# Sparse attention before two mixtures of experts: units of scores taken two by two, probabilities transposed a slot later, four buffers for them

## The chip, the cores and the metric

The kernel runs on one core of a Trainium2 chip. The metric is the device time of one execution in microseconds (us). Matrix work is done by TensorE (PE, with its weight loads listed as PEld), element-wise work by VectorE (DVE) and ScalarE (ACT), a little by GpSimd (POOL); SyncE (SP) issues most of the DMAs. PE writes only into PSUM (`ps`, eight banks of 512 float32 per partition), and DVE or ACT take results out of there.

## The reference, cut to what matters

Two batches, eight heads, 768 positions, head size 64. A position sees 8 global keys and the 96 keys up to itself, with a bias that falls with the distance. Behind it come a routed MoE (8 experts) and a dense one (4 experts).

```python
scores = scale * np.matmul(q, k.transpose(0, 1, 3, 2))
keep = is_global | is_local
bias = -slopes[:, None, None] * dist[None, :, :]
scores = np.where(keep, scores + bias, -1e9)
a = np.exp(scores - np.max(scores, axis=-1, keepdims=True))
a = a / (np.sum(a, axis=-1, keepdims=True) + 1e-09)
x = np.matmul(a, v)                       # then as (1536, 512)
# moe: rows with x @ w_skip > 0 go to expert argmax(x @ w_gate), others pass
# moe2: out = sum over e of p[:, e] * (relu(x @ w1[e]) @ w2[e])
```

## The kernel before, in words

The attention stage is the first 141 us. It has eight blocks `n` (`NB`; a pair of heads in one batch) of six units (`NI`; a tile of 128 queries), 48 units `u` in all. A query tile needs 256 keys: its own tile and a window made of the previous tile's last 96 keys and the first 32 keys of all; tile 0 needs its own 128 only and is the narrow unit. Each engine runs a program of its own, written out in order, and semaphores tie them; nothing is scheduled by a planner. So what stands behind a wait on its engine waits too.

For a unit the steps are these.

- `scores(u)` on PE: three products (high and low parts of float32 numbers, in fp32r), each for both heads, whose 64 rows lie in the two halves of the array. The result is in banks 0 and 1. It counts up `s_done`.
- `masked(u)` on DVE (L1080): adds the bias and takes the row's extreme, one instruction a head, into `p_sb` (one of three buffers) and `nmax`. `sm_done`.
- `exps(u)` on ACT (L805): the exponential in place, one a head. `ex_done`.
- `probs_T(u)` on PE (L1581): four transposes into bank 2 or 3. `pt_tr`.
- `probs_out(u)`: the copy of the transposed tile to SBUF, on ACT (L811) for tiles 1, 3 and 4 of a block (`by_act`), on DVE (L1089) for the others.
- `pv(u)` on PE (L1596, L1597): four float32 products with V and a column of ones, into bank 4 or 5. `pv_done`.

Beside the units a block has: four fills, which transpose keys and queries of the next block (`fill`, L1552) and of which ACT takes the high part (`keys_high`, `queries_high`, L785 and L791) and DVE the low part (`keys_low`, `queries_low`, L1058 and L1063); POOL's `windows`, which puts the key windows together (`kw_done`); `normalise` on DVE (L1096 to L1103), twice a block, for three tiles each; `outputs_T` on PE (L1605), which transposes the normalised outputs; `xo_out` on ACT (L797), their copy; `logits` on PE (L1613), their product with the router's weights; and `add_logits` on DVE (L1109).

In unit `u` PE's order is: scores(u), a fill for the next block, probs_T(u-1), in two units outputs_T, in two others logits, and pv(u-2). The logits of a half stand one unit behind the outputs_T of that half. The masks of unit `u` are made while PE transposes unit `u-1`. The fills and the transposed outputs share banks 6 and 7 in turn (`groups`, `group_bank`, `group_out`).

The stages behind the attention are not touched: routing, the first MoE (L1748), and the second (L1844 and L1867), which fills the last two thirds of the time. They start from the last addition of logits.

## Time and profile before

| | us |
|---|---|
| median of three runs | 780.96 (780.90 to 781.52) |
| the profiled execution, its own time | 780.86 |
| its span, first to last instruction | 779.1 |
| PE busy in the span | 752.0 (97%) |
| DVE busy | 471.3 (60%) |
| ACT busy | 328.7 (42%) |

The span is what the profiler sees from the first to the last instruction; the time lies 1.76 us above it. A timeline row gives start, duration, engine, source line, operation, output and inputs with their shapes, and how many instructions were merged in it; in brackets the idle time of the engine before it and what ended it. Merged rows of weight loads overlap each other, so starts tell more than durations. "issue" names idle time that no other engine is seen to end.

### The profile page before, as it was taken

The numbers are of one execution on the slowest core, as the hardware profiler recorded it, in microseconds if no ns is written. First come the engines' busy times: TensorE is split into PE (matmuls) and PEld (weight loads), VectorE is DVE, ScalarE is ACT, GpSimd is POOL, SyncE is SP. The second block draws the span as 40 slices with busy tenths as digits, with TensorE's granted clock in tenths as the row PEclk, the third lists the DMA queues.
The fourth block names the chain that finished last, engine by engine and source line by source line (L and its number), as shares of the span: only waits on it lengthen the run. The fifth ranks groups of instructions, "written<-read, shape, count | busy, mean of one in ns | idle before, by whom it ended". The sixth has DMA issues, their size and how long they took to land.

```text
span 779.1 us, 11259 instructions
## 1 busy us (share of the span) xinstructions
PE 752.0 (97%) x4199; PEld 671.5 (86%) x4199; DVE 471.3 (60%) x924; ACT 328.7 (42%) x586; POOL 42.0 (5%) x86
## 2 busy tenths in 40 slices
PE   3999999699999999999999999999999999999998
PEld 2889889488888988998989989989899899898896
DVE  5766666699888398554474375275365365456442
ACT  2566566388988263431422233234144053143230
POOL 3100100110100320000000000000000000000000
PEclk9999999699999999999999999999999999999999
DMA  9469970599990530020011011002003002000112
GB/s 151 100 151 263 274 218 21 204 393 389 390 389 25 163 117 5 1 109 0 1 55 55 1 54 55 1 4 105 0 0 108 0 0 109 0 0 0 40 40 81
DMA packets 86944, 79.28 MB, mean 102 GB/s; under 512 B 50802, under 2 KB 56948, under 8 KB 86900
## 3 DMA queue, kind: packets, MB, share of 16 engines
q1 hardware_dynamic: 81540, 71.32, 28.9%
q0 software_dynamic: 1600, 5.24, 2.1%
q10 hardware_dynamic: 3760, 2.14, 0.9%
q8 instruction: 26, 0.43, 0.2%
q14 instruction: 18, 0.15, 0.1%
HBM read 70.30 MB, written 8.39 MB: 101 GB/s over the span
## 4 chain that ended last, share of the span: by engine, by line
PE 91%; DVE 6%; DMA 1%; ACT 1%; issue 1%; POOL 0%; DVEq 0%; SPq 0%
PE ps L1867 32%; PE ps L1844 29%; PE ps L1748 11%; PE ps L1572 3%; PE ps L1597 2%; PE ps L1596 2%; PE ps L1581 2%; PE ps L1552 2%; PE ps L1799 1%; PE ps L1613 1%; PE ps L1804 1%; PE ps L1605 1%; PE ps L1723 1%; DVE xs L1441 1%; DVE X L1103 1%
## 5 line engine op out<-in xcount | busy, mean ns | idle before, releaser
L1867 PE MATMUL ps<-w2s,h_hi 128*128 128x512 f32 x768 | 237.1, 390 | 0.4 <-DVE X L1479 0.4
L1844 PE MATMUL ps<-xs,w1s 128*128 128x384 f32 x1344 | 236.6, 335 | 0.7 <-ACT xs L941 0.7
L1844 PEld LDWEIGHTS ps<-xs,w1s 128*128 128x128 f32 x1344 | 233.8, 188 | 2.2 <-ACT xs L941 0.9
L1867 PEld LDWEIGHTS ps<-w2s,h_hi 128*128 128x128 f32 x768 | 143.8, 188 | 29.9 <-DVE X L1479 0.8
L1867 PE MATMUL ps<-w2s,h_lo 128*128 128x512 f32 x384 | 149.8, 390 | 0.0
L1481 DVE SCALAR_TENSOR_TENSOR X<-ps,prn,X 128x512 f32<-128x512 f32 x84 | 63.1, 751 | 121.7 <-PE ps L1867 121.3
L951 ACT ACTIVATE shared<-ps 128x384 f32<-128x384 f32 x96 | 46.1, 488 | 156.2 <-PE ps L1844 156.0
L1450 DVE TENSOR_TENSOR shared<-ps,shared 128x384 f32<-128x384 f32 x96 | 53.3, 557 | 92.4 <-PE ps L1844 92.1
L1867 PEld LDWEIGHTS ps<-w2s,h_lo 128*128 128x128 f32 x384 | 72.1, 188 | 15.1
L954 ACT ACTIVATE h_hi<-shared 128x384 fp32r<-128x384 f32 x96 | 50.4, 526 | 67.8 <-DVE shared L1450 67.8
L1021 DVE TENSOR_TENSOR piece_lo<-ring,piece_hi 128x1024 fp32r<-128x1024 f32 x48 | 56.4, 1219 | 5.5 <-ACT piece_hi L773 5.4
L1080 DVE CUSTOM_DVE_ANT_0 area<-ps,shared 128x256 f32<-128x256 f32 (+1 forms) x96 | 34.8, 399 | 31.2 <-PE ps L1572 30.1
L1456 DVE SCALAR_TENSOR_TENSOR h_lo<-shared,h_hi 128x384 fp32r<-128x384 f32 x96 | 50.2, 551 | 2.0
L805 ACT ACTIVATE area<-area,shared 128x256 f32<-128x256 f32 (+1 forms) x96 | 41.6, 481 | 21.3 <-DVE shared L1080 21.3
L773 ACT ACTIVATE piece_hi<-ring 128x1024 fp32r<-128x1024 f32 x48 | 47.9, 1053 | 1.9 <-ACT area L888 1.9
L870 ACT ACTIVATE w2s<-raw 128x1024 fp32r<-128x1024 f32 x16 | 16.1, 1053 | 70.4 <-PE ps L1867 70.4
L1748 PE MATMUL ps<-piece_hi,xT_r 128*128 128x512 f32 x128 | 35.8, 402 | 0.8 <-ACT xT_r L883 0.8
L1597 PE MATMUL ps<-X,raw 128*128 128x65 f32 x192 | 35.8, 276 | 0.0
L1748 PE MATMUL ps<-piece_hi,hT_r 128*128 128x512 f32 x128 | 35.0, 396 | 0.0
L1596 PE MATMUL ps<-X,raw 128*128 128x65 f32 x160 | 30.0, 269 | 0.0
L1597 PEld LDWEIGHTS ps<-X,raw 128*128 128x128 f32 x192 | 28.9, 195 | 0.0
L1581 PE MATMUL ps<-ident,area 128*128 128x128 f32 x176 | 28.9, 284 | 0.0
(183 smaller groups left out, 819.5 us busy)
## 6 DMA issues: line engine op xcount, KB each, us to landing
ring<-in_moe_w SPq DMA_DIRECT2D x24, 1024.0 KB, 12.0
raw<-in_moe_w SPq DMA_DIRECT2D x16, 1024.0 KB, 5.1
shared<-in_moe_w SPq DMA_DIRECT2D x8, 1024.0 KB, 10.3
X<-in_k SPq DMA_DIRECT2D x16, 192.0 KB, 4.2
shared<-in_q SPq DMA_DIRECT2D x16, 192.0 KB, 4.3
X<-in_v SPq DMA_DIRECT2D x16, 192.0 KB, 2.9
x_d<-X SPq DMA_DIRECT2D x8, 384.0 KB, 3.2
X<-x_d SPq DMA_DIRECT2D x2, 1536.0 KB, 16.3
```

The costliest lines, as they stand in the source:

```text
L773: act.activation(unit(piece_hi[b % NHI], x), unit(piece_raw[b % NR], x), ACT.Copy).then_inc(p_hi, 1)
L951: act.activation(part[:, slot, f, :], ps[:, 3 * f + BANK[ITEMS[item][0]], 0:HT], ACT.Copy).then_inc(copied, 1)
L954: act.activation(h_hi[:, c, second * HT:second * HT + HT], src, ACT.Relu).then_inc(hd_hi, 1)
L1021: dve.tensor_tensor(unit(piece_lo[b % NR], x), unit(piece_raw[b % NR], x), unit(piece_hi[b % NHI], x).bitcast(F32), ALU.subtract).then_inc ...
L1450: dve.tensor_tensor(part[:, slot, f, :], ps[:, 3 * f + BANK[ITEMS[item][0]], 0:HT], part[:, slot, f, :], ALU.add).then_inc(added, 1)
L1456: dve.scalar_tensor_tensor(h_lo[c][:, here], src, 0.0, h_hi[:, c, here].bitcast(F32), ALU.max, ALU.subtract).then_inc(hd_lo, 1)
L1481: dve.scalar_tensor_tensor(X[:, t, :], ps[:, 6 + k % 2, :], p_, X[:, t, :], ALU.mult, ALU.add).then_inc(acc_done, 1)
L1596: pe.matmul(out_, pt_sb[u % 3][:, 2 * h, :], prev, start=True, stop=False)
L1597: mm = pe.matmul(out_, pt_sb[u % 3][:, 2 * h + 1, :], vn[b][:, i, h, :], start=(i == 0), stop=True)
L1748: mm = pe.matmul(ps[:, bank, :], src[xp][:, c0 + c, :], w[wp][:, c, :], start=(x == 0 and c == 0 and not (kind == "B" and half)), stop=(x ...
L1844: mm = pe.matmul(out_, w1s[:, wp, WI[name], c, f * P:(f + 1) * P], xs[:, 3 * b:3 * b + 3, xp, XI[name], c, :], start=(not onto and x == 0 ...
L1867: mm = pe.matmul(ps[:, 6 + k % 2, :], h_, w2s[:, wp, c, :], start=(x == 0 and c == 0), stop=(x == 2 and c == 3))
```

## The change

The program on PE, ACT and DVE goes by slots of two units `u` and `u+1`, three slots `s` a block. PE computes the scores of both one after the other; the second unit's result lies in the other half of banks 0 and 1 (`off`). Transposes of the probabilities are those of the slot before, as are their copies; P·V follows with unit `u-3` and `u-2`. There are four buffers of `p_sb` and `nmax`. `by_act` now means even units. Both fills of keys stand in slot 0, both fills of queries in slot 1. outputs_T of a block's first half and its xo_out stand in slot 0 of the next block and their logits in slot 1; outputs_T of the second half, its xo_out and its logits all stand in slot 2. The wait for `kw_done` moves from tile 0 to tile 1. DVE begins the masks of a slot when both scores are there, except in the first slot. `probs_T` and the index of `p_sb` in it change from `u % 3` to `u % 4` as in the other places. SP and POOL keep their programs.

Two places show what moves. The first is on PE, in the third block: around outputs_T of the second half (L1605, now L1615) of the block before. Scores are L1572, now L1582; probs_T L1581, now L1591; P·V L1596 and L1597, now L1606 and L1607; logits L1613, now L1623. Before:

```order
L1605 MATMUL ps<-ident,X 128x128 [waits o_done,q_lo]
L1605 MATMUL ps<-ident,X 128x128 x2
L1596 MATMUL ps<-X,raw 128x65 [waits pt_act]
L1597 MATMUL ps<-X,raw 128x65
L1596 MATMUL ps<-X,raw 128x65
L1597 MATMUL ps<-X,raw 128x65
L1572 MATMUL ps<-kh_52,qh_54 128x256 [waits sm_done,q_lo]
L1572 MATMUL ps<-kh_52,qh_54 128x256
L1572 MATMUL ps<-kh_52,ql_55 128x256 x2
L1572 MATMUL ps<-kl_53,qh_54 128x256 x2
L1581 MATMUL ps<-ident,area 128x128 [waits pt_act,ex_done]
L1581 MATMUL ps<-ident,area 128x128 x3
```

Now, from the last scores of slot 2 on:

```order
L1582 MATMUL ps<-kl_53,qh_54 128x256 x2
L1615 MATMUL ps<-ident,X 128x128 [waits o_done,q_lo]
L1615 MATMUL ps<-ident,X 128x128 x2
L1591 MATMUL ps<-ident,area 128x128 [waits pt_act,ex_done]
L1591 MATMUL ps<-ident,area 128x128 x3
L1606 MATMUL ps<-X,raw 128x65 [waits pt_dve]
L1607 MATMUL ps<-X,raw 128x65
L1606 MATMUL ps<-X,raw 128x65
L1607 MATMUL ps<-X,raw 128x65
L1591 MATMUL ps<-ident,area 128x128 [waits pt_dve,ex_done]
L1591 MATMUL ps<-ident,area 128x128 x3
L1623 MATMUL ps<-wg,area 128x9 [waits xo_cp]
```

outputs_T had the four transposes of probabilities in front of it and now comes first behind the scores. Before, the logits of that half followed behind the next unit's scores and transposes (just below the piece); now they stand in the same slot as their outputs_T.

The second place is on DVE, in the same block, tiles 2 and 3: queries_low (L1063, now L1069), normalise (L1096 to L1103, now L1102 to L1109), masked (L1080, now L1086) and probs_out (L1089, now L1095). Before:

```order
L1063 SCALAR_TENSOR_TENSOR ql_59<-ps,qh_58 128x512 [waits q_hi]
L1096 TENSOR_SCALAR shared<-ps 128x6 [waits pv_done]
L1098 RECIPROCAL shared<-shared 128x6 [waits o_step]
L1103 TENSOR_TENSOR X<-ps,shared 128x384 [waits o_step]
L1080 ISA area,shared<-ps,shared 128x256 [waits pt_tr,s_done]
L1080 ISA shared 128x1
L1080 ISA area,shared<-ps,shared 128x256
L1080 ISA shared 128x1
L1063 SCALAR_TENSOR_TENSOR ql_59<-ps,qh_58 128x256 [waits q_hi]
L1089 COPY raw<-ps 128x512 [waits pv_done,pt_tr]
```

Now:

```order
L1069 SCALAR_TENSOR_TENSOR ql_59<-ps,qh_58 128x512 [waits q_hi]
L1086 ISA area,shared<-ps,shared 128x256 [waits pt_tr,s_done]
L1086 ISA shared 128x1
L1086 ISA area,shared<-ps,shared 128x256
L1086 ISA shared 128x1
L1095 COPY raw<-ps 128x512 [waits pv_done,pt_tr]
L1069 SCALAR_TENSOR_TENSOR ql_59<-ps,qh_58 128x256 [waits q_hi]
L1102 TENSOR_SCALAR shared<-ps 128x6 [waits pv_done]
L1104 RECIPROCAL shared<-shared 128x6 [waits o_step]
L1109 TENSOR_TENSOR X<-ps,shared 128x384 [waits o_step]
```

normalise stood behind the first queries_low, ahead of masked for tile 3; it now stands behind that mask, a probs_out and the second queries_low.

```diff
@@ -157,10 +157,10 @@
             ql.append(take_r(f"ql{b}", NI, P))
         qn = [take(NI, 2 * D) for _ in range(2)]
         nbias = take(H, BW)
-        nmax = take(6)
+        nmax = take(8)
         rsum = take(6)
         rinv = take(6)
-        p_sb = [at(work, 512 * j, (4, P), "") for j in range(3)]
+        p_sb = [at(work, 512 * j, (4, P), "") for j in range(4)]
         Xf = X[:, :, :].rearrange("p t d -> p (t d)")
         vn = [at(Xf, 780 * b, (NI, 2, VW), "") for b in range(2)]
@@ -477,17 +477,19 @@
         NU_ = NB * NI
+        NS = NI // 2
         LG = 400
         FIRST = ["k0", "k1", "q0", "q1"]
-        FILL = FIRST + [None, None]
         groups = [(0, g) for g in FIRST]
         for n_ in range(NB):
-            for i_ in range(NI):
-                if n_ + 1 < NB and FILL[i_]:
-                    groups.append((n_ + 1, FILL[i_]))
-                if n_ and i_ in (0, 3):
-                    groups.append((n_ - 1, "xa" if i_ == 0 else "xb"))
+            for s_ in range(NS):
+                if n_ + 1 < NB and s_ < 2:
+                    groups += [(n_ + 1, g) for g in FIRST[2 * s_:2 * s_ + 2]]
+                if n_ and s_ != 1:
+                    groups.append((n_ - 1, "xb" if s_ else "xa"))
         groups += [(NB - 1, "xa"), (NB - 1, "xb")]
         place = {g: j for j, g in enumerate(groups)}
@@ -508,7 +510,7 @@
         def by_act(u):
-            return u % NI in (1, 3, 4)
+            return u % 2 == 0
         def pt_count(u):
@@ -801,8 +803,8 @@
                 c0 = 1 if u % NI == 0 else 0
                 for h in range(2):
                     act.wait_ge(sm_done, 2 * u + h + 1)
-                    part = p_sb[u % 3][:, 2 * h + c0:2 * h + 2, :]
-                    act.activation(part, part, ACT.Exp, bias=nmax[:, u % 3 * 2 + h:u % 3 * 2 + h + 1], scale=-1.0).then_inc(ex_done, 1)
+                    part = p_sb[u % 4][:, 2 * h + c0:2 * h + 2, :]
+                    act.activation(part, part, ACT.Exp, bias=nmax[:, u % 4 * 2 + h:u % 4 * 2 + h + 1], scale=-1.0).then_inc(ex_done, 1)
             def probs_out(u):
                 c0 = 1 if u % NI == 0 else 0
@@ -816,22 +818,26 @@
                     keys_high(0, c)
                 for c in range(2):
                     queries_high(0, c)
-                for u in range(NU_):
-                    n, i = u // NI, u % NI
-                    if n + 1 < NB and i < 4:
-                        if i < 2:
-                            keys_high(n + 1, i)
-                        else:
-                            queries_high(n + 1, i - 2)
+                for u in range(0, NU_, 2):
+                    n, s = u // NI, u % NI // 2
+                    high = (keys_high, queries_high, None)[s] if n + 1 < NB else None
+                    if high:
+                        high(n + 1, 0)
+                    if u:
+                        probs_out(u - 2)
                     exps(u)
-                    if n and i in (0, 3):
-                        xo_out(n - 1, i // 3)
-                    if u and by_act(u - 1):
-                        probs_out(u - 1)
-                    if n == NB - 1 and i < 2:
+                    if high:
+                        high(n + 1, 1)
+                    if n and s == 2:
+                        xo_out(n - 1, 1)
+                    exps(u + 1)
+                    if n and s == 0:
+                        xo_out(n - 1, 0)
+                    if n == NB - 1 and s < 2:
                         act.wait_ge(s_done, NI * (NB - 1))
                         piece_loaded(act, 0)
-                        piece_high(0, i)
+                        piece_high(0, s)
+                probs_out(NU_ - 2)
                 xo_out(NB - 1, 0)
                 xo_out(NB - 1, 1)
             with act.Else():
@@ -1073,14 +1079,14 @@
                     if i == 0 and n % 2 == 0:
                         dve.wait_ge(setup, 10 + 2 * (n // 2) + h)
                     if h == 0:
-                        dve.wait_ge(s_done, u + 1)
-                        wait(dve, pt_tr, u - 2)
+                        dve.wait_ge(s_done, u + 1 if u < 2 else u // 2 * 2 + 2)
+                        wait(dve, pt_tr, u - 3)
                     head = 2 * (n // 2) + h
                     lo = ONE if i == 0 else PREV
-                    dve.tensor_tensor_reduce(p_sb[u % 3][:, 2 * h + c0:2 * h + 2, :].rearrange("p a k -> p (a k)"),
-                                             ps[:, h, c0 * P:2 * P], nbias[:, head, lo:lo + (2 - c0) * P],
+                    dve.tensor_tensor_reduce(p_sb[u % 4][:, 2 * h + c0:2 * h + 2, :].rearrange("p a k -> p (a k)"),
+                                             ps[:, h, (u % 2 * 2 + c0) * P:(u % 2 * 2 + 2) * P], nbias[:, head, lo:lo + (2 - c0) * P],
                                              1.0, BIG, ALU.add, ALU.min,
-                                             accum_out=nmax[:, u % 3 * 2 + h:u % 3 * 2 + h + 1]).then_inc(sm_done, 1)
+                                             accum_out=nmax[:, u % 4 * 2 + h:u % 4 * 2 + h + 1]).then_inc(sm_done, 1)
             def probs_out(u):
                 c0 = 1 if u % NI == 0 else 0
@@ -1126,27 +1132,30 @@
                     queries_low(0, c)
                 for h in range(2):
                     head_bias(h)
-                for u in range(NU_):
-                    n, i = u // NI, u % NI
+                for u in range(0, NU_, 2):
+                    n, s = u // NI, u % NI // 2
+                    low = (keys_low, queries_low, None)[s] if n + 1 < NB else None
+                    if n and s == 0:
+                        normalise(n - 1, 0)
+                        if n > 1:
+                            add_logits(n - 2)
                     masked(u)
-                    if n + 1 < NB and i < 4:
-                        if i < 2:
-                            keys_low(n + 1, i)
-                        else:
-                            queries_low(n + 1, i - 2)
-                    if u and not by_act(u - 1):
+                    if low:
+                        low(n + 1, 0)
+                    masked(u + 1)
+                    if u:
                         probs_out(u - 1)
-                    if n and i == 2:
+                    if low:
+                        low(n + 1, 1)
+                    if n and s == 1:
                         normalise(n - 1, 1)
-                    if i == 5:
-                        normalise(n, 0)
-                        if n:
-                            add_logits(n - 1)
-                    if n == 0 and 2 + i < H:
-                        head_bias(2 + i)
+                    if n == 0:
+                        head_bias(2 + 2 * s)
+                        head_bias(3 + 2 * s)
+                normalise(NB - 1, 0)
+                add_logits(NB - 2)
                 unit_low(0, 0)
-                if not by_act(NU_ - 1):
-                    probs_out(NU_ - 1)
+                probs_out(NU_ - 1)
                 unit_low(0, 1)
                 normalise(NB - 1, 1)
                 add_logits(NB - 1)
@@ -1561,15 +1570,16 @@
             def scores(u):
                 n, i = u // NI, u % NI
                 b, c0 = n % 2, 1 if i == 0 else 0
-                if i == 0:
+                if i == 1:
                     pe.wait_ge(kw_done, 4 * n + 4)
                 if i in (0, 4):
                     pe.wait_ge(q_lo, 2 * n + i // 4 + 1)
-                wait(pe, sm_done, 2 * u)
+                wait(pe, sm_done, 2 * u if u < 2 else u // 2 * 4)
+                off = u % 2 * 2 * P
                 for x, (qt, kt) in enumerate(((qh, kh), (ql, kh), (qh, kl))):
                     for h in range(2):
                         r = slice(D * h, D * h + D)
-                        mm = pe.matmul(ps[:, h, c0 * P:2 * P], qt[b][r, i, :], kt[b][r, i, c0 * P:2 * P], start=(x == 0), stop=(x == 2))
+                        mm = pe.matmul(ps[:, h, off + c0 * P:off + 2 * P], qt[b][r, i, :], kt[b][r, i, c0 * P:2 * P], start=(x == 0), stop=(x == 2))
                 mm.then_inc(s_done, 1)
             def probs_T(u):
@@ -1618,21 +1628,33 @@
                 for g in FIRST:
                     fill(0, g)
                 pe.wait_ge(v_ones, 4)
-                for u in range(NU_):
-                    n, i = u // NI, u % NI
+                for u in range(0, NU_, 2):
+                    n, s = u // NI, u % NI // 2
                     scores(u)
-                    if n + 1 < NB and FILL[i]:
-                        fill(n + 1, FILL[i])
-                    if u >= 1:
+                    scores(u + 1)
+                    if n + 1 < NB and s < 2:
+                        for g in FIRST[2 * s:2 * s + 2]:
+                            fill(n + 1, g)
+                    if n and s == 1:
+                        logits(n - 1, 0)
+                    if n and s == 2:
+                        outputs_T(n - 1, 1)
+                    if u:
+                        probs_T(u - 2)
+                    if u >= 4:
+                        pv(u - 3)
+                    if u:
                         probs_T(u - 1)
-                    if n and i in (0, 3):
-                        outputs_T(n - 1, i // 3)
-                    if n and i in (1, 4):
-                        logits(n - 1, i // 3)
-                    if u >= 2:
+                    if n and s == 0:
+                        outputs_T(n - 1, 0)
+                    if n and s == 2:
+                        logits(n - 1, 1)
+                    if u:
                         pv(u - 2)
+                probs_T(NU_ - 2)
+                pv(NU_ - 3)
+                probs_T(NU_ - 1)
                 outputs_T(NB - 1, 0)
-                probs_T(NU_ - 1)
                 pv(NU_ - 2)
                 logits(NB - 1, 0)
                 pv(NU_ - 1)
```

## Rows read from the trace of the kernel before

**Rows 1.** Stages: stretch, length, busy us (instructions) by engine, PEclk, DMA share, GB/s.

```profile
60.00:80.00 20.00, 19.79 (x182) 18.11 (x182) 13.82 (x53) 12.52 (x31) 1.82 (x5) 1.00 0.95 278
...
136.00:138.00 2.00, 0.83 (x8) 0.73 (x7) 1.07 (x4) 0.00 (x0) 0.00 (x0) 0.93 0.00 0
138.00:140.00 2.00, 1.42 (x7) 1.02 (x6) 0.00 (x0) 0.49 (x1) 0.00 (x0) 0.50 0.62 191
```

**Rows 2.** Timeline, weight loads at two block beginnings: start, us, engine, line, what, count.

```profile
75.23 0.19 PEld L1572 LDWEIGHTS ps<-kh,qh 64*128 64x128 f32 x2
...
90.05 0.19 PEld L1572 LDWEIGHTS ps<-kh,qh 64*128 64x128 f32 x2
...
90.53 0.20 PEld L1552 LDWEIGHTS ps<-ident,X 128*128 128x128 f32 x2
```

**Rows 3.** Waits of the weight loads, 30 to 119 us: total, times, longest.

```profile
PEld ps L1605 <- issue: 2.5, 6, 0.4
```

**Rows 4.** Timeline, weight loads from 95 to 99 us.

```profile
95.00 0.30 PEld L1597 LDWEIGHTS ps<-X,raw 128*128 128x128 f32 x2
95.37 0.19 PEld L1572 LDWEIGHTS ps<-kh,qh 64*128 64x128 f32 x2
...
95.59 0.19 PEld L1572 LDWEIGHTS ps<-kl,qh 64*128 64x128 f32 x2
95.92 0.42 PEld L1552 LDWEIGHTS ps<-ident,shared 128*128 128x128 f32 x4
96.31 0.47 PEld L1581 LDWEIGHTS ps<-ident,area 128*128 128x128 f32 x4
...
98.94 0.31 PEld L1605 LDWEIGHTS ps<-ident,X 128*128 128x128 f32 x3 [0.42 <-issue]
```

**Rows 5.** Timeline, VectorE from 97 to 100 us.

```profile
97.24 0.69 DVE L1063 SCALAR_TENSOR_TENSOR ql<-ps,qh 128x512 fp32r<-128x512 f32 x1 [0.43 <-ACT qh L791]
97.85 0.15 DVE L1096 TENSOR_SCALAR shared<-ps 128x6 f32<-128x6 f32 x1
...
98.26 0.56 DVE L1103 TENSOR_TENSOR X<-ps,shared 128x384 f32<-128x384 f32 x1
...
99.08 0.42 DVE L1080 CUSTOM_DVE_ANT_0 area<-ps,shared 128x256 f32<-128x256 f32 x1
...
99.42 0.42 DVE L1063 SCALAR_TENSOR_TENSOR ql<-ps,qh 128x256 fp32r<-128x256 f32 x1
99.76 0.68 DVE L1089 COPY raw<-ps 128x512 f32<-128x512 f32 x1
```

**Rows 6.** Timeline, ScalarE from 96 to 99 us.

```profile
96.61 0.60 ACT L791 ACTIVATE qh<-ps 128x512 fp32r<-128x512 f32 x1 [1.69 <-PE ps L1552]
97.11 0.90 ACT L805 ACTIVATE area<-area,shared 128x256 f32<-128x256 f32 x2
97.91 0.58 ACT L811 ACTIVATE raw<-ps 128x512 f32<-128x512 f32 x1
98.38 0.38 ACT L791 ACTIVATE qh<-ps 128x256 fp32r<-128x256 f32 x1
```

**Rows 7.** Timeline at the end of the attention, ScalarE and weight loads.

```profile
138.76 0.49 ACT L797 ACTIVATE area<-ps 128x384 f32<-128x384 f32 x1 [4.39 <-PE ps L1605]
...
139.30 0.29 PEld L1613 LDWEIGHTS ps<-wg,area 128*128 128x128 f32 x1 [0.98 <-ACT area L797]
```

**Rows 8.** Timeline, a weight load and VectorE, last units of the attention.

```profile
133.29 0.31 PEld L1605 LDWEIGHTS ps<-ident,X 128*128 128x128 f32 x3 [0.54 <-issue]
...
140.79 0.21 DVE L1109 TENSOR_TENSOR lg<-ps,lg 128x54 f32<-128x54 f32 x1 [3.09 <-PE ps L1613]
```

**Rows 9.** Timeline, weight loads in the first block.

```profile
18.04 0.29 PEld L1572 LDWEIGHTS ps<-kh,qh 64*128 64x128 f32 x2 [0.33 <-DVE shared L1080]
...
18.98 0.29 PEld L1552 LDWEIGHTS ps<-ident,X 128*128 128x128 f32 x2 [0.22 <-issue]
...
20.67 0.29 PEld L1572 LDWEIGHTS ps<-kh,qh 64*128 64x128 f32 x2 [0.98 <-DVE shared L1080]
```

More of the change, by code:

```diff
@@ L1580, in probs_T @@
                     if u % NI or x % 2:
-                        mm = pe.transpose(ps[:, 2 + u % 2, x * P:(x + 1) * P], p_sb[u % 3][:, x, :], ident[:, :])
+                        mm = pe.transpose(ps[:, 2 + u % 2, x * P:(x + 1) * P], p_sb[u % 4][:, x, :], ident[:, :])
                 mm.then_inc(pt_tr, 1)
```

## The prediction

> **What bounds the kernel now.** I read the page first, then the stages, then the attention stage instruction by instruction, since the change touches nothing behind it. In a stretch of 20 us inside the attention TensorE (PE) is busy 19.79 us, VectorE (DVE) 13.82 and ScalarE (ACT) 12.52, at the full granted clock [rows 1]. So attention is bound by PE's own instructions, and nearly everything it waits for comes in time.
>
> The attention runs over eight blocks (a pair of heads of one batch each) of six units (query tiles). A block begins with the narrow scores of tile 0; two such beginnings stand at 75.23 and 90.05, so a block takes 14.82 us [rows 2]. The last addition of logits, the end of the attention, is at 140.79 [rows 8]. What stands behind it (routing, first MoE, second MoE) starts from there and is the same program, so what the attention gains or loses goes into the total one for one.
>
> Inside a block the only regular wait of PE is the one before L1605, the transposes of the normalised outputs: 2.5 us of weight-load idle in six waits between 30 and 119 us, 0.42 us each [rows 3]. The second cost that a reader should see is not called a wait anywhere: it is the edge between scores and everything else. Loads of one kind follow each other every 0.11 us: two of P·V, 0.19 each, fill 0.30 together from 95.00, so the last of them starts at 95.11. The first scores' load stands at 95.37, 0.26 behind it; the pairs of scores' loads follow at 0.11 (95.37 to the third pair at 95.59), and the next kind's load stands at 95.92, 0.33 behind. The four transposes there fill 0.42 where the next four fill 0.47 [rows 4]. So an entry into scores costs 0.15 us more than a regular step, and an exit some 0.20 less the 0.05 given back: 0.30 us for the edges of one unit. A narrow unit takes 0.48 to the next kind instead of 0.55 [rows 2, 4], so I give it 0.25.
>
> **The change part by part.** A slot is now two units. (1) The scores of both follow each other, so one exit and one entry in each pair go: two pairs of wide units at 0.30 and one with the narrow unit at 0.25, 0.85 us a block and 6.8 over eight. This price isn't in the trace, since no two units stand side by side; inside a unit, though, the three pairs of loads follow at 0.11 [rows 4], and the second unit's six loads are of the same kind, so I take the full 0.30. The other end is nothing gained.
> The Trainium skill bears on just this ("TensorEngine Tiling (Array Packing)", Key Properties): changing the tiling mode drains the array, changing the tile within a mode does not. By that rule the gain is the 6.8 us; a reading in which each unit drains would give 0.
>
> (2) Matmuls, transposes, evacuations, exps and DMAs are as many as before. The fourth buffer of p_sb lies in free space and lets the DVE run one slot ahead. On SP and POOL nothing moves; its loads are issued as before relative to the blocks, whole blocks ahead of their use, so I cost them at nothing.
>
> (3) What the order does to the wait before L1605. I follow slot 1 of a block (tiles 2 and 3), with time 0 at its first scores' load. PE: six pairs of scores' loads and the exit 0.90, six transposes of the queries 0.60, six loads of logits 0.67, two transposes of the narrow unit 0.22, P·V 0.89, four transposes 0.44, narrow P·V 0.45, entry 0.15: slot 2 starts at 4.31. Its own scores take 0.90, so outputs_T (before L1605), which now stands directly behind them, is ready at 5.21.
> ACT takes the first four transposed queries 0.69 after their first load (95.92 to 96.61 [rows 4, 6]), so at 1.59, and needs 0.60. DVE starts queries_low at 2.22 and goes on 0.61 later (97.24 to 97.85) at 2.83. Then come masked(u+1), twice 0.34 (99.08 to 99.42), to 3.52; probs_out(u-1), which must wait for transposes that start at 3.28, so 3.99 (0.69 and a little, as for ACT), and 0.61 (97.24 to 97.85 is of the same size) to 4.60; the second queries_low 0.34 (99.42 to 99.76), to 4.94; and normalise, 97.85 to 98.82, 0.97, to 5.91 [rows 5]. PE sees it 0.12 later (98.82 to 98.94 [rows 4, 5]), at 6.03. So PE waits 0.82 us where it lost 0.40 before (the idle 0.42, and 0.03 by which loads otherwise overlap, less a first step that is 0.05 shorter). Before, normalise stood in front of masked of tile 3 and outputs_T behind four transposes; now it is the last thing of the DVE's slot, and outputs_T comes first behind the scores. Term: +0.42 a block.
>
> (4) A new wait, before logits (L1613) of the second half, which now stand in the same slot as their outputs_T. On ACT xo_out is queued behind probs_out(u-2) and exps(u). With outputs_T at 6.03, transposes of the probabilities start at 6.30, ACT copies from 7.00 (0.69 again), goes on after 0.47 (97.91 to 98.38), then two exps 0.80 (97.11 to 97.91) [rows 6] and xo_out 0.49, to 8.76; PE gets it 0.05 later (138.76 + 0.49 to 139.30 [rows 7]), at 8.81. PE's own work in front (transposes 0.44, P·V 0.89, transposes 0.44) ends at 8.07. Term: +0.74. The wait has no cover: before, the logits stood a whole unit behind their outputs_T, with a P·V and a unit of scores between. Behind PE's wait stand one P·V and the next slot's scores, and on them everything else.
> Both waits run through ACT and DVE chains of six or so instructions; if each hand-over is 0.05 us off, the two together move by some 0.3. I keep 0.6 to 1.7 for their sum over before, and take 1.16.
>
> Steady block: -0.85 + 0.42 + 0.74 = +0.31, with rounding 0.3 to 0.4. Over blocks 1 to 6: +2.0.
>
> (5) Block 0 has no outputs, so it lacks both waits, and scores(0) no longer waits for POOL's windows (only tile 1 does). But it runs at the half clock, where loads take twice as long, and scores(2) must wait for masked(1), which sits on DVE behind keys_low(1,0); PE already waited 0.98 for such a thing [rows 9]. I put that at +1.4 against 0.85 of edges: +0.5, between -1.0 and +2.0.
> (6) Block 7 has no fills: edges -0.85, the new waits about +1.2, before's own waits there (0.54 before L1605 at 133.29 [rows 8], and two short ones) fall away, about -0.9. The last chain, normalise, outputs_T, xo_out, logits, is in both. -0.5, between -1.5 and +1.0.
>
> **Sum.** 2.0 + 0.5 - 0.5 = +2.0 us on the profiled execution, whose own time is 780.86 us (span 779.1, 1.76 around it); it is 0.1 below the median 780.96. Forecast 782.9 us.
>
> **The rivals.**
> *The clock falls at the new waits.* What speaks for it: at the end of the attention PE is busy 0.83 of 2 us, and in the next 2 us the granted clock is 0.50 [rows 1], the level of 1.2 GHz; the new waits are 0.8 and 0.7, in thin work, three microseconds apart. Against it: the wait of 0.54 at 133.29 [rows 8] passed without a fall, and between the waits PE is busy. At the half clock loads come every 0.22 instead of 0.11 (the scores' unit at 18.04 takes 0.94 to the next kind, not 0.55) [rows 9]; the rest of such a slot, some 3 us, would take up to 3 more. In one or two of the six blocks: +2 to +5, 785 to 788. Chance 0.17.
> The Trainium skill warns of it in "TensorE: Matmul & The Clock Gate", "A second HAM failure mode": short idles between groups make the clock swing. The full clock with waits of 0.42 in every block [rows 1, 3] says it doesn't happen at that size; no row shows it at twice the size.
> *Merging the scores buys nothing.* Each unit drains even beside another: 6.8 us come back, 789.7. The 0.11 between different tiles of a unit speaks against it. Chance 0.07.
> *Only one new wait is real* (the other side). The place is ACT's order in slot 2: if xo_out is through 0.7 us sooner than by my chain, logits run unhindered, and a block is at -0.43; it decides at a total of 0.85 for both waits over before. Seven blocks without 0.74: 777.7. For it: ACT has the time, 12.5 of 20 us [rows 1]. Against: it is an order and not a load, and each link has its row. Chance 0.11.
> *Both waits are hidden.* -6.8 and some of the old wait: 774. It would need DVE to reach normalise by 4.1 instead of 4.94. Chance 0.05.
>
> **How the numbers follow.** Forecast case 0.60, own range 781.3 to 784.7 (the bounds of (3) to (6) added as independent). What a measurement can tell from no change is 0.2%, 1.6 us: faster is under 779.4, slower over 782.5. Of the forecast case 0.17 lies below 782.5 and 0.43 above. Faster: 0.11 + 0.05 = 0.16. Same: 0.17. Slower: 0.43 + 0.17 + 0.07 = 0.67. The range of 8 in 10 takes in the one-wait case and the clock case to 787.5, and leaves out both-hidden and nothing-bought: 777.0 to 787.5.
>
> **What would show each step.** Weight loads of twelve scores in a row at 0.11, and one exit a slot: (1). A block of about 15.15 us between narrow scores, not 14.82. PE's wait before the outputs' transposes released by DVE's normalise, about 0.8 us, in blocks 1 to 6; a second, of 0.7 to 0.8, before the second logits of a block, released by ACT's xo_out: (3), (4). Granted clock 1.00 from about 25 us to the end of the attention. The last addition of logits near 142.8. I am wrong if the block is shorter than 14.82, if one of the waits is missing, if the clock shows halves in mid-attention, or if the difference arises behind the attention.

## The result and the profile after

The changed kernel takes 794.02 us (median of four, 793.38 to 795.50), the kernel before 781.17 in the same comparison: a ratio of 1.016 with a 95% interval of 1.012 to 1.020. The forecast was 782.9 us. The profiled execution took 793.38 us with a span of 791.6, 12.5 us more than the 779.1 of before. Its mean granted clock is 0.972 to 0.976 in all four executions; the kernel before has 0.985 to 0.993 in every one that was taken. Here and below a ratio leaves out executions that lie over 1.5% above the fastest of their kernel, which are a few of the kernel before near 792 us and two of the four of paused_before.

I read the end of the attention first. The last addition of logits stood at 140.79 [rows 8]; now:

```profile
153.50 0.21 DVE L1115 TENSOR_TENSOR lg<-ps,lg 128x54 f32<-128x54 f32 x1 [2.16 <-PE ps L1623]
```

It is 12.7 us late. Behind it come 638.1 us to the end of the span, and 638.3 before. So the whole difference arises in the attention. Then the beginnings of blocks, which answer to [rows 2] (weight loads of the narrow scores):

```profile
29.90 0.19 PEld L1582 LDWEIGHTS ps<-kh,qh 64*128 64x128 f32 x2
...
45.00 0.19 PEld L1582 LDWEIGHTS ps<-kh,qh 64*128 64x128 f32 x2
...
60.09 0.19 PEld L1582 LDWEIGHTS ps<-kh,qh 64*128 64x128 f32 x2
...
76.84 0.19 PEld L1582 LDWEIGHTS ps<-kh,qh 64*128 64x128 f32 x2
...
93.57 0.19 PEld L1582 LDWEIGHTS ps<-kh,qh 64*128 64x128 f32 x2
...
108.67 0.19 PEld L1582 LDWEIGHTS ps<-kh,qh 64*128 64x128 f32 x2
...
125.37 0.18 PEld L1582 LDWEIGHTS ps<-kh,qh 64*128 64x128 f32 x2
```

Blocks 1, 2 and 5 take 15.10 us, where 15.15 was forecast. Blocks 3, 4 and 6 take 16.7, and the last one 28.1 to the last addition, against 21.10 before. There are two kinds of blocks, and the stages say what parts them. Columns as in [rows 1]; the one that answers to it is the first:

```profile
60.00:80.00 20.00, 18.63 (x159) 17.54 (x159) 12.20 (x48) 9.52 (x23) 1.66 (x4) 0.87 0.85 232
58.00:61.00 3.00, 2.61 (x27) 2.41 (x27) 1.27 (x4) 1.13 (x3) 0.00 (x0) 1.00 0.86 198
61.20:64.40 3.20, 3.20 (x17) 3.20 (x16) 1.90 (x10) 1.63 (x4) 0.00 (x0) 0.50 0.93 269
64.60:78.00 13.40, 12.03 (x118) 11.14 (x118) 8.06 (x30) 6.89 (x17) 1.66 (x4) 1.00 0.84 237
...
126.00:142.80 16.80, 16.80 (x93) 15.89 (x91) 6.92 (x31) 6.86 (x15) 0.00 (x0) 0.50 0.08 24
143.20:153.00 9.80, 7.90 (x69) 7.32 (x68) 5.50 (x11) 3.21 (x8) 0.00 (x0) 1.00 0.06 20
```

The granted clock falls to 0.50, the level of 1.2 GHz, for 3.4 us at 61.1, 78.1 and 108.9, and for 17.1 us from 125.9 to 143.0. Before, it stayed full from 25.1 to 137.7. A reader who looks only at busy shares sees nothing: PE is busy 16.80 of 16.80 us in the worst stretch. The number of instructions tells (93 in 16.8 us, where a full-clock stretch of 13.4 us has 118).

What stands just ahead of each fall is slot 2 of a block, where the two forecast waits are; the clock goes down 1.9 to 3.0 us behind the end of the second. Timeline, the counterpart of [rows 4, 5]: start, us, engine, line, what, count, idle before it and what ended it:

```profile
53.80 0.19 PEld L1582 LDWEIGHTS ps<-kh,qh 64*128 64x128 f32 x2
53.91 0.19 PEld L1582 LDWEIGHTS ps<-kh,ql 64*128 64x128 f32 x2
54.03 0.19 PEld L1582 LDWEIGHTS ps<-kl,qh 64*128 64x128 f32 x2
54.15 0.19 PEld L1582 LDWEIGHTS ps<-kh,qh 64*128 64x128 f32 x2
54.27 0.19 PEld L1582 LDWEIGHTS ps<-kh,ql 64*128 64x128 f32 x2
54.39 0.19 PEld L1582 LDWEIGHTS ps<-kl,qh 64*128 64x128 f32 x2
...
54.87 0.56 DVE L1109 TENSOR_TENSOR X<-ps,shared 128x384 f32<-128x384 f32 x1
...
55.54 0.31 PEld L1615 LDWEIGHTS ps<-ident,X 128*128 128x128 f32 x3 [0.97 <-DVE ql L1069]
55.57 0.52 PE L1615 MATMUL ps<-ident,X 128*128 128x128 f32 x3 [0.79 <-DVE X L1109]
...
57.86 0.48 ACT L799 ACTIVATE area<-ps 128x384 f32<-128x384 f32 x1
...
58.39 0.74 PEld L1623 LDWEIGHTS ps<-wg,area 128*128 128x128 f32 x6 [0.81 <-ACT area L799]
58.39 0.84 PE L1623 MATMUL ps<-wg,area 128*128 128x9 f32 x6 [0.57 <-ACT area L799]
```

Six pairs of scores' loads follow at 0.11 to 0.12, then the first wait ends with normalise and the second with xo_out. Counted as in the prediction, the first is 55.54 - 53.80 less 0.90 of scores, 0.84 us (0.82 was forecast), and the second is 58.39 - 55.54 less 2.04 of PE's own work, 0.81 us (0.74 forecast). The idle of the weight loads, by which the two are named below, is 0.97 and 0.81. The sums answer to [rows 3] (30 to 119 us; total, times, longest):

```profile
PEld ps L1615 <- DVE ql L1069: 4.8, 5, 1.0
PEld ps L1623 <- ACT area L799: 4.1, 5, 0.8
```

The ledger of the 12.7 us: block 1 begins 0.9 earlier (29.90 for 30.77); six blocks at +0.28 are 1.7; three falls are 4.9 (16.75 + 16.73 + 16.70 - 3 x 15.10); the last block is 7.0.

Which blocks lose the clock is not fixed. Two kernels below, fill_6 and refill_7, have both pauses whole in blocks 1 to 5. In their profiled executions the clock falls near the starts of blocks 2, 3, 4 and 5 and of blocks 2, 4, 5, 6 and 7; here it falls near those of blocks 3, 4, 6 and 7.

### The profile page after: what moved, and what is told of

Read it like the earlier page. It is cut to its first block, busy times and chain, and to the rows that moved or that the text cites. A ratio compares the mean times of both kernels' runs of the same rounds, so it can differ in the third digit from the quotient of the medians.

```text
span 791.6 us, 11266 instructions
## 1 busy us (share of the span) xinstructions
PE 757.2 (96%) x4199; PEld 680.7 (86%) x4199; DVE 473.1 (60%) x924; ACT 326.5 (41%) x586; POOL 42.3 (5%) x86
## 4 chain that ended last, share of the span: by engine, by line
PE 90%; DVE 6%; ACT 2%; issue 1%; DMA 1%; DVEq 0%; SPq 0%; ACTq 0%
PE ps L1889 32%; PE ps L1866 29%; PE ps L1770 11%; PE ps L1591 3%; PE ps L1582 2%; PE ps L1607 2%; PE ps L1606 2%; PE ps L1561 2%; PE ps L1623 2%; PE ps L1821 1%; PE ps L1826 1%; PE ps L1615 1%; PE ps L1745 1%; ACT area L807 1%; DVE xs L1450 1%
## 5 line engine op out<-in xcount | busy, mean ns | idle before, releaser
L1086 DVE CUSTOM_DVE_ANT_0 area<-ps,shared 128x256 f32<-128x256 f32 (+1 forms) x96 | 33.8, 397 | 11.0 <-PE ps L1582 10.2
L1607 PE MATMUL ps<-X,raw 128*128 128x65 f32 x192 | 38.8, 294 | 0.0
L1607 PEld LDWEIGHTS ps<-X,raw 128*128 128x128 f32 x192 | 31.9, 213 | 0.1
L1606 PE MATMUL ps<-X,raw 128*128 128x65 f32 x160 | 32.0, 284 | 0.0
L1591 PE MATMUL ps<-ident,area 128*128 128x128 f32 x176 | 31.6, 306 | 0.0
```

Source lines behind the costliest of these rows:

```text
L1591: mm = pe.transpose(ps[:, 2 + u % 2, x * P:(x + 1) * P], p_sb[u % 4][:, x, :], ident[:, :])
L1607: mm = pe.matmul(out_, pt_sb[u % 3][:, 2 * h + 1, :], vn[b][:, i, h, :], start=(i == 0), stop=True)
```

## The experiments

Two theories stood against each other. A: the two pauses of PE in slot 2 let the clock fall. B: the order does it, since it puts all the scores of a slot together and leaves long stretches of thin work. Ratios are to the kernel before, with their 95% intervals; each kernel was executed four or ten times, and one execution of it was profiled. Line numbers differ a little from kernel to kernel. "First pause" is the one ahead of the outputs' transposes, "second pause" the one ahead of the second half's logits.

### The pauses taken away by place: no_waits, first_gone, second_gone

```diff
                     if n and s == 1:
                         logits(n - 1, 0)
-                    if n and s == 2:
-                        outputs_T(n - 1, 1)
+                    if n > 1 and s == 0:
+                        pe.wait_ge(o_done, 2 * n - 1)
+                        logits(n - 2, 1)
                     if u:
                         probs_T(u - 2)
                     if u >= 4:
                         pv(u - 3)
+                    if n and s == 2:
+                        outputs_T(n - 1, 1)
...
-                    if n and s == 2:
-                        logits(n - 1, 1)
```

On DVE add_logits(n - 2) goes to slot 1, and the last of those logits stand behind the last block's outputs_T. first_gone has only the move of outputs_T, second_gone only that of the logits.

> The changed kernel with both new waits taken away by place: in slot 2 the transposes of the second half's outputs stand behind the transposes and the P.V of a unit, and that half's logits go to slot 0 of the next block (their addition on VectorE to slot 1). All scores stay in pairs. Theory A (the two pauses of PE in slot 2 let the clock fall): without them a block takes about 13.6 us (15.10 less 0.8 and 0.7), the granted clock stays 1.00 to the last few us of the attention, the last addition of logits is near 133, and the time is 772 to 775. Theory B (the clock falls because the paired order leaves long stretches of thin transposes and P.V without scores between them, pauses or not): blocks of 13.6 at the full clock, but again three or four falls with 1.6 us each and a slow last block, 778 to 786. If merging the scores had bought nothing, a block would take some 14.5 and the time would be 779 or more.

> Only the transposes of the second half's outputs are moved, behind the first P.V of slot 2; its logits stay at the end of the same slot. By the chain of durations PE then waits nothing before the transposes and about 0.45 us before the logits, and a block takes about 14.1 us. Theory A: one pause of 0.45 is as small as the 0.42 in every block of the kernel before, so the clock stays full: last addition of logits near 135, time 774 to 777. Theory B: falls as in the changed kernel, 781 to 788.

> Only the logits of the second half are moved, to slot 0 of the next block; the transposes of its outputs stay directly behind the scores of slot 2, with their pause of some 0.8 us. A block takes about 14.4 us at the full clock. Theory A in its strict form (both pauses, three microseconds apart, are needed): clock full, last addition of logits near 138, time 777 to 780. Theory A in its loose form (one pause of 0.8 is enough): falls of 1.6 us in some blocks, 781 to 788. Theory B: falls as well, 782 to 790.

Measured: 771.28 us (0.989, 0.986 to 0.991), 773.75 (0.9915, 0.989 to 0.994) and 778.17 (0.996, 0.995 to 0.9975). Blocks take 13.38, 13.94 and 14.22 us. The attention of no_waits in one row:

```profile
26.00:128.00 102.00, 100.49 (x989) 95.81 (x985) 76.15 (x285) 64.02 (x153) 9.88 (x24) 1.00 0.70 181
```

None of the three has a fall in blocks 1 to 6. All three ended within or under the times that theory A gave, since their blocks are 0.2 us shorter than I had expected. second_gone keeps the first pause whole (0.97 in blocks 1 to 6), and first_gone keeps 0.49 of the second. This is theory A; but moving things changes the order too, so it is not proof against B.

### The pauses filled where they stand: filled, fill_first, fill_second, fill_half, wide_first

```diff
+            def busy(bank, k):
+                for _ in range(k):
+                    pe.transpose(ps[:, bank, 0:P], ident[:, :], ident[:, :])
...
                     if n and s == 2:
+                        pe.wait_ge(pt_sem(u - 4), pt_count(u - 4))
+                        busy(2, 8)
                         outputs_T(n - 1, 1)
...
                     if n and s == 2:
+                        pe.wait_ge(pt_sem(u - 2), pt_count(u - 2))
+                        busy(2, 6)
                         logits(n - 1, 1)
```

filled has 8 and 6 such transposes, fill_first 8 and 0, fill_second 0 and 6, fill_half 0 and 3; wide_first has seven pairs of `pe.matmul(ps[:, 2 + h, 0:2 * P], qh[b][r, i, :], kh[b][r, i, 0:2 * P])` in the first place and nothing in the second. Where the count is 0 the added wait still stands; in fill_first the second pause is then 0.88 and not 0.81.

> The changed order word for word, but while PE would wait it transposes the identity into a free half of bank 2: 8 transposes before those of the outputs, 6 before the second logits, in each block from 1 to 7. They are of no use and take 0.11 us each, so a block takes about 15.2 us at the full clock, where the changed kernel takes 15.10. Theory A: the clock stays 1.00 up to the last chain, the last addition of logits is near 143 and the time is 782 to 785, some 10 us less than the changed kernel although PE does more. Theory B: the falls stay where they are and the time is 793 to 797.

> The changed order with 8 useless transposes in the first pause only, before the transposes of the outputs; PE still waits some 0.8 us before the second logits. Without falls the time is 782 to 783. If both pauses are needed for a fall (as the kernel with only the outputs' pause left suggests) the clock stays full to the last chain: 781.5 to 783.5. If a single pause of 0.8 in this order is enough: falls of 1.6 us each and a slow last block, 785 to 794.

> The changed order with 6 useless transposes in the second pause only; PE still waits some 0.8 to 1.0 us before the transposes of the outputs. Both needed: full clock, 781.5 to 783.5. One enough: 785 to 794. If the two kernels with one pause filled differ from each other, the place of the pause matters and not only its size.

> The changed order with the first pause filled by 14 products like those of the scores (64 rows, 256 columns, fp32r, seven pairs at 0.11 us) instead of 8 transposes; the second pause stays. With transposes in this place the clock still fell. Theory E (what fills the pause matters; transposes keep PE busy but not its clock): no fall, block 15.1 to 15.3, 782 to 784. Theory C (only the second pause decides): falls as in the changed kernel, 789 to 800.

> The changed order with 3 useless transposes in the second pause, which leaves some 0.5 us of it; the first pause of 0.97 stays. Without falls the time is 780.5 to 783. If the size of the second pause decides and 0.5 is below it (as in the kernel with only the outputs' transposes moved, whose pause of 0.49 let nothing fall, though with no first pause): 780.5 to 783. If the two pauses add up: some falls, 783 to 792.

Measured, in the same order: 782.08 (1.002, 1.001 to 1.003), 796.43 (1.020, 1.014 to 1.026), 780.86 (1.000, 0.998 to 1.002), 795.41 (1.018, 1.015 to 1.021) and 781.65 (0.9997, 0.997 to 1.002). B is refuted: the order of the useful work is the changed one word for word, PE does more work, and filled is 12 us faster than the changed kernel. The two with one pause filled part by 16 us; fill_first ended above both of its forecasts, fill_second under both. In fill_second the first pause stands as before, and the clock is full to the last chain:

```profile
26.00:141.00 115.00, 107.88 (x1036) 101.65 (x1033) 75.74 (x286) 64.76 (x155) 9.92 (x24) 1.00 0.61 165
```

The same holds in fill_half:

```profile
55.28 0.31 PEld L1615 LDWEIGHTS ps<-ident,X 128*128 128x128 f32 x3 [0.97 <-issue]
...
58.13 0.74 PEld L1623 LDWEIGHTS ps<-wg,area 128*128 128x128 f32 x6 [0.48 <-ACT area L799]
58.13 0.84 PE L1623 MATMUL ps<-wg,area 128*128 128x9 f32 x6 [0.25 <-ACT area L799]
```

That is a first pause of 0.97 and a second of 0.48, and the clock is 1.00 until 139.0. All ten executions of fill_second and of fill_half have a mean granted clock of 0.989 to 0.993, as the kernel before; the four of fill_first 0.966 to 0.974, the four of wide_first 0.970 to 0.978. With the second pause whole, as in wide_first, it falls four times, whatever fills the first:

```profile
58.20 0.74 PEld L1623 LDWEIGHTS ps<-wg,area 128*128 128x128 f32 x6 [0.81 <-ACT area L799]
```

And its last stretch at the half clock:

```profile
125.60:142.40 16.80, 16.80 (x100) 15.89 (x99) 7.03 (x32) 6.33 (x13) 0.00 (x0) 0.50 0.08 23
```

So in this order it is the second pause, and at 0.8 us but not at 0.5. In fill_half the three transposes shorten the pause and also add work, which this run can't tell apart; first_gone, with 0.49 and no useless work (but without the first pause, and in another order), keeps the clock too. Nor is it the sum of the two: fill_half has 1.45 us and no fall, fill_first 0.88 and four. My strict form of A, that both are needed, fell with fill_first. Nor was it the kind of filler: theory E fell with wide_first.

### The same pauses in the order before: paused_before, before_first, before_second

```diff
+                for n in range(NB):
+                    if n + 1 < NB:
+                        windows(n + 1)
+                    for x, k in enumerate((2, 1) if n else ()):
+                        pool.wait_ge(pt_tr, NI * n + 3 + x)
+                        for y in range(k):
+                            steps += 1
+                            pool.memset(zrow[:, :], 0.0).then_inc(paced, 1)
+                            pool.wait_ge(paced, steps)
...
+                    if n and i in (3, 4):
+                        pe.wait_ge(paced, 3 * n - (0 if i == 4 else 1))
```

before_first and before_second have one of the two.

> The kernel before in its own order, with two pauses of PE put into each block from 1 to 7, about where the changed kernel has them, three microseconds apart: PE waits before the transposes of the second half's outputs until GpSimd has filled 256 zeros twice after the fourth transposes of the block, and one unit later before the logits until it has done so once. By the rows of GpSimd (0.30 us a fill) PE's weight loads should stand still some 1.0 and 0.8 us instead of 0.42 and nothing, and a block takes about 15.8 us at the full clock, for 787 us in all if the clock stays. Theory A, in general form (two such pauses near each other let the clock fall in any order of work): falls in some blocks, 790 to 800. Theory A', that it needs the paired order's thin work around the pauses as well: no fall before the end of the attention, 786 to 788.

> The kernel before with only the first of the two pauses of 'paused_before' (PE's weight loads stand still 1.0 us instead of 0.42 before the transposes of the second half's outputs). At the full clock a block takes 15.2 to 15.4 us and the time is 784 to 785. Theory C (it is the second pause, amid logits and P.V with no scores beside it, that lets the clock fall, or only with it): no fall inside the attention. Theory D (in this order any pause of 1 us is enough, since PE works less densely around it): half-clock stretches again, 790 to 830.

> The kernel before with only the second pause (PE's weight loads stand still 0.7 us before the logits of the second half, where they waited for nothing; the pause of 0.42 stays). At the full clock a block takes about 15.4 us and the time is 785 to 786. Theory C: half-clock stretches as with both pauses, 800 to 830. Theory that the sum of both must pass some size: this one falls less often than both together (sum 1.1 against 1.7 us), 785 to 800.

Measured: paused_before took 816.19, 823.99, 844.13 and 844.22 us (median 834.06; the ratio of 1.051, 1.044 to 1.057, goes by the lower two, 820.1 on average); before_first 784.86 (1.005, 1.004 to 1.007) and before_second 792.34 (1.016, 1.010 to 1.021; 787.52 to 796.04 in its four executions). Timeline of paused_before (the profiled execution, 844 us):

```profile
119.29 0.31 PEld L1616 LDWEIGHTS ps<-ident,X 128*128 128x128 f32 x3 [1.01 <-POOL zrow L721]
...
122.29 0.74 PEld L1624 LDWEIGHTS ps<-wg,area 128*128 128x128 f32 x6 [0.71 <-POOL zrow L721]
```

Three of its stretches:

```profile
60.00:74.80 14.80, 14.80 (x76) 13.65 (x75) 6.39 (x24) 4.96 (x12) 1.64 (x4) 0.50 0.21 49
...
113.00:139.00 26.00, 23.49 (x208) 20.77 (x206) 15.95 (x62) 14.88 (x35) 5.11 (x14) 1.00 0.76 195
140.00:156.80 16.80, 16.80 (x86) 15.54 (x86) 6.16 (x25) 5.11 (x12) 1.65 (x4) 0.50 0.38 129
```

The pauses have the sizes meant, and here most falls last 17 us or more instead of 3.4, so that four of the blocks 1 to 6 take 24 us. Theory A gave 790 to 800; even the lower two executions lie 16 to 24 us above that, with mean granted clocks of 0.952 and 0.944, under every other kernel's here. In the profiled one the falls are only a part: its loads of scores are still 0.21 to 0.22 apart just before 51 us (52 matmuls from 30 to 40 us, where the kernel before has 91), so the clock came up some 26 us later than in the kernel before. That began before the first added pause and cost 4.7 us in block 0 alone; why it did so is open. before_first, with its pause of 1.0 in every block, has none:

```profile
27.00:145.00 118.00, 110.23 (x990) 99.61 (x988) 74.14 (x284) 67.72 (x154) 14.15 (x38) 1.00 0.60 162
```

before_second has one of 6.8 us before its last chain in its profiled execution (789.5 us, below the median), at 106.1, behind its pause of 0.66 at 104.3; the other five in blocks 1 to 6, of the same size, let nothing fall:

```profile
107.00:112.80 5.80, 5.80 (x31) 5.56 (x30) 2.92 (x13) 2.56 (x6) 0.00 (x0) 0.50 0.73 276
```

Theory C gave it 800 to 830 and missed; 792 lies where the theory of the two pauses' sum had put it. In this order the runs don't exclude that theory: before_first has 1.0 us in all and no fall, before_second 0.42 and 0.66 and one. Together with the paired order they fit the second pause as the one that lets the clock fall, the first alone doing nothing; but here the first adds to the second (816 or more against 796 or less), which it didn't in the paired order.

### The last block: fill_1to6, fill_6, refill_7

fill_1to6 is filled without its transposes in block 7; fill_6 has six in the second pause of block 6 alone; refill_7 is the changed kernel with six where block 7 has no fills:

```diff
+                    if n + 1 == NB and s < 2:
+                        pe.wait_ge(pt_sem(u - 4), pt_count(u - 4))
+                        busy(2, 6)
```

> Both pauses filled in blocks 1 to 6, none in block 7, which has no fills of keys and queries. This gives the price of the last block by itself. If block 7 alone (its pauses, and its thin work) loses the clock, it starts at the full clock near 120.4, falls behind its second slot and ends 1 to 5 us later than with block 7 filled: 783 to 787. If the 17 us at the half clock in the changed kernel were a consequence of the fall just before it, block 7 runs at the full clock here: 782 to 783.

> The changed kernel with 6 useless transposes in the second pause of block 6 alone. The falls at the starts of blocks 3, 4 and 6 stay (1.6 us each). If the 17 us at the half clock in block 7 come from that one pause at the end of block 6, the last block runs at the full clock to its last chain and the time is 785 to 788, some 7 us under the changed kernel. If block 7 falls by itself once the clock has fallen before: 792 to 795.

> The changed kernel with 6 useless transposes in slot 0 and 6 in slot 1 of block 7, where the other blocks have their fills. At the full clock they cost 1.3 us, at the half clock 2.6. If the missing fills are what keeps the clock down, it comes back after 3.4 to 6.8 us instead of 17: 788 to 791. If transposes do nothing for the clock: 795.5 to 797.

Measured: 782.37 us (1.0025, 1.001 to 1.004), 788.02 (1.009, 1.0065 to 1.012) and 788.58 (1.009, 1.007 to 1.012). Stretches of fill_6:

```profile
44.80:48.00 3.20, 3.20 (x20) 2.98 (x19) 1.89 (x8) 0.65 (x2) 0.00 (x0) 0.50 0.61 119
...
99.40:147.00 47.60, 42.45 (x405) 39.78 (x403) 29.70 (x107) 25.26 (x58) 3.30 (x8) 1.00 0.43 129
```

Its last addition of logits:

```profile
148.13 0.21 DVE L1115 TENSOR_TENSOR lg<-ps,lg 128x54 f32<-128x54 f32 x1 [2.54 <-PE ps L1623]
```

Stretches of refill_7:

```profile
127.30:130.60 3.30, 3.30 (x19) 3.30 (x18) 1.12 (x9) 1.37 (x4) 0.00 (x0) 0.50 0.03 5
131.00:147.00 16.00, 14.96 (x142) 14.17 (x139) 9.63 (x29) 8.21 (x17) 0.00 (x0) 1.00 0.09 26
```

fill_6 still falls in the middle of the attention (four times 3.4 us, in other blocks than I had expected), but six useless transposes at the end of block 6 keep the last block at the full clock: it begins at 126.48, so it takes 21.65 us, not 28.13. All ten executions of fill_6 (786.68 to 791.36) lie under all four of the changed kernel (793.38 to 795.50). In fill_1to6 the clock is full until 139.8, and it is 0.3 us above filled: block 7 loses next to nothing by its own pauses; it pays for the last one before it. refill_7 falls at the start of block 7 as the changed kernel does, and is back after 3.4 us instead of 17: twelve useless transposes save 5 us. So where the last block starts at the half clock, work in the place of the fills that it lacks brings the clock back sooner. Missing fills are not the whole of it: in paused_before falls of 17 us lie in blocks that have theirs.

### The edges of scores: split

```diff
                     scores(u)
+                    if n + 1 < NB and s < 2:
+                        fill(n + 1, FIRST[2 * s])
                     scores(u + 1)
                     if n + 1 < NB and s < 2:
-                        for g in FIRST[2 * s:2 * s + 2]:
-                            fill(n + 1, g)
+                        fill(n + 1, FIRST[2 * s + 1])
```

> The kernel with both pauses taken away ('no_waits', 771.28 us, blocks of 13.38), with one fill of keys or queries between the two units of scores in slots 0 and 1; nothing else is moved. This puts back two of the three exits and entries of scores that a block saved. By the prediction's term (0.25 with the narrow unit, 0.30 between wide ones) a block takes 13.9 us and seven blocks with fills cost 3.9 us: 774.5 to 775.5. If merging had bought nothing: 771.3. The clock should stay full in both cases.

Measured: 773.93 us (0.992, 0.991 to 0.994), blocks of 14.02 us against 13.38. Two edges put back cost 0.64 us; the forecast was 0.55. No wait of more than 0.2 us came with them.

## Why the prediction was wrong

**The terms of the sum held within their bounds.** (1) An edge of scores is worth 0.32 us (split), where I took 0.25 to 0.30; over the 24 pairs of units that is 7.7 us, an estimate from split, for my 6.8. (3), (4) The waits came with their places, their releasers and nearly their sizes, and the steady block is 15.10 us for 15.15. (5) Block 1 begins 0.9 us earlier, where +0.5 was forecast between -1.0 and +2.0. The first scores no longer wait for the windows and start at 14.38 instead of 16.13; the next units then pay part of it back:

```profile
16.45 0.32 PEld L1582 LDWEIGHTS ps<-kh,qh 64*128 64x128 f32 x2 [1.33 <-POOL kl L706]
...
20.63 0.29 PEld L1582 LDWEIGHTS ps<-kh,qh 64*128 64x128 f32 x2 [2.07 <-DVE shared L1086]
```

In other executions of kernels that are the same up to there (fill_6, refill_7) block 1 begins at 29.11, so 0.8 us of this term change from one execution to the next. (6) At the full clock block 7 takes 21.65 us (fill_6) against 21.10: +0.55 for my -0.5, inside its bounds. The errors of (5) and (6), -1.4 and +1.05, nearly cancel, which is luck. The range of 781.3 to 784.7 was too narrow for its own terms: (3) and (4) alone, with 0.55 either way in each of six like blocks, are 3.3 us either way. Fill_half, the changed order with nothing of its path lengthened and the second pause at 0.5 us, takes 781.65 us: that is what the sum was about, 1.3 below the forecast.

**The step that failed** is "Granted clock 1.00 from about 25 us to the end of the attention", on which the forecast stood, and the rival that denied it got 0.17 and a price of 2 to 5 us for "one or two of the six blocks". The clock was a term of nothing in the sum. Three falls cost 4.9 us (1.6 each), and the fourth, in the last block, about 6.5 (28.13 less 21.65): 11.4 of the 12.7. The mechanism was named; its chance, its number and its price in the last block were wrong, and I kept it out of the sum.

Three things in my working of that rival were wrong. First, the argument against it: "the wait of 0.54 at 133.29 [rows 8] passed without a fall", and the 0.42 in every block. Both stand in the place of the first pause, which before_first shows harmless at 1.0 us; they said nothing of a pause amid logits, transposes and P.V. Second, the new waits are in every block, and I still counted one or two falls; there were four. Third, I ended its price with the slot in which it happens. The last block has no fills, and a fall at its start lasted 17 us, for half of the whole loss.

The Trainium skill's warning, in "TensorE: Matmul & The Clock Gate", "A second HAM failure mode", which I had set aside for want of a row, describes, for another kernel, short idles between groups of matmuls and a clock that swings between its levels. The runs here agree with it in kind: a pause of 0.8 us at one place is enough, one of 0.97 at another is not.

**What is shown and what is not.** Shown: the second pause causes the falls (filled and fill_second against fill_first and wide_first); with 0.5 us of it left there are none (fill_half, first_gone); the first alone causes none, in either order (fill_second, before_first); the length of the last fall hangs on the work that follows it (refill_7). Not shown: whether filling helps by the shorter pause or by the work added; why the place matters. The second pause lies between thin products, the first follows scores or stands just ahead of them; that is a fact of the order and no proof. Nor do the runs say why falls last 3.4 us (once 6.8) inside the paired order and mostly 17 in paused_before, nor why the same pauses at the ends of blocks 1 and 4 of the changed kernel let nothing fall here, while in the profiled execution of refill_7, the same program up to block 7, those two let the clock fall and that of block 2 did not.

## What to carry to other kernels

A new wait of TensorE can have two prices: its length, and what the clock does after it. The second can be by far the larger: here the new order with all its waits costs 1.3 us, and the clock 11.4. So a wait amid thin work should be filled or moved, even with useless transposes, before the reorder that made it is judged; a few of them, as many as fit into the pause, turned 794 into 781 (fill_second). And once its two waits are moved away (no_waits, 771.28 us, 0.989 of the kernel before), the same pairing of units is faster than both kernels.

## What the runs showed that I had not expected

- Two pauses of 1.0 and 0.7 us in seven blocks, 12 us at most by their own length, came with 35 to 63 us more (paused_before; part of it, in the profiled execution, is the late start of the full clock). The last stretch at 0.50 lasts 51 us, from 163.7 to 214.9; the last addition of logits stands at 204.17 in it.
- PE can be busy 16.80 of 16.80 us and stay at the half clock all the while (126.0 to 142.8), and in refill_7 be back after 3.30 of 3.30. Busy share doesn't tell the two apart.
- 14 wide products more in each block, in the first pause, changed nothing in the number of falls (wide_first, four; 795.4 us against 794.0).
